# The weighing's last tile of 64 keys a head: one fp32 product, or three products of split fp32r halves

## The reference

```python
def _attn_ref(q, k, v, cap):
    scores = np.matmul(q, k.transpose(0, 1, 3, 2)) / np.sqrt(q.shape[-1])
    scores = cap * np.tanh(scores / cap)
    attn = np.exp(scores - np.max(scores, axis=-1, keepdims=True))
    attn = attn / (np.sum(attn, axis=-1, keepdims=True) + 1e-09)
    return np.matmul(attn, v)

h = x @ w_in
x = np.maximum(0.01 * h, h) @ w_out
xn = x / np.sqrt(np.mean(x * x, axis=-1, keepdims=True) + 1e-06) * rms_g
g = xn @ w_gate
out = (g / (1 + np.exp(-g)) * (xn @ w_val)) @ w_out2
```

## Time and profile before

| what | value |
|---|---|
| runs before (3) | 567.91 us median, 567.53 to 568.76 |
| the profiled execution's own time | 568.21 us |
| its span | 566.4 us |
| TensorE busy | 561.6 us (99%) |
| VectorE busy | 413.7 us (73%) |
| ScalarE busy | 294.4 us (52%) |
| GpSimd busy | 313.8 us (55%) |

### The profile page before, as it was taken

One profiled execution on the slowest core, in us unless ns is written; L12 is line 12 of the kernel. 1 busy time (PEld: TensorE's weight loads), 2 busy tenths in 40 slices (PEclk: granted clock), 3 DMA queues, 4 the chain that ended last, 5 costly groups with the idle time before them and its releaser, 6 DMA issues.

```text
span 566.4 us, 7857 instructions
## 1 busy us (share of the span) xinstructions
PE 561.6 (99%) x2706; PEld 472.0 (83%) x2706; DVE 413.7 (73%) x575; ACT 294.4 (52%) x513; POOL 313.8 (55%) x272
## 2 busy tenths in 40 slices
PE   9999999999999999999999999999999999999997
PEld 5544554688999999999999999999999999998896
DVE  4468897685545455324985499999999999999963
ACT  6889888226444464434644456444334445825330
POOL 1026464479656652234853469767766897526672
PEclk9999999999999999999999999999999999999999
DMA  6355332123111142110211011111221111120511
GB/s 171 97 174 162 110 113 52 49 57 112 57 56 57 56 130 66 57 45 23 75 54 57 1 57 57 56 57 56 77 89 59 56 57 58 56 57 0 171 73 65
DMA packets 29720, 41.49 MB, mean 73 GB/s; under 512 B 17009, under 2 KB 18673, under 8 KB 29681
## 3 DMA queue, kind: packets, MB, share of 16 engines
q1 hardware_dynamic: 29536, 40.99, 23.0%
q10 hardware_dynamic: 144, 0.00, 0.0%
HBM read 38.15 MB, written 2.80 MB: 72 GB/s over the span
## 4 chain that ended last, share of the span: by engine, by line
PE 91%; DVE 4%; issue 3%; DMA 1%; ACT 0%; POOL 0%; DVEq 0%; ACTq 0%
PE ps L1579 46%; PE ps L1646 21%; PE ps L1514 9%; PE ps L1743 8%; PE ps L1502 4%; PE ps L1520 2%; PE ps L1506 1%; DVE act_lo L1321 1%; DVE x_lo L1321 1%; PE ps L1588 1%; DMA sums<-x_raw 1%; DVE x_raw L955 0%; DVE s_sum L1024 0%; POOL w_lo L576 0%; PE ps L1698 0%
## 5 line engine op out<-in xcount | busy, mean ns | idle before, releaser
L576 POOL TENSOR_TENSOR w_lo<-w_raw,w_hi 128x384 fp32r<-128x384 f32 x111 | 131.1, 1189 | 140.3 <-ACT w_hi L686 139.6
L1579 PE MATMUL ps<-x_hi,w_hi 128*128 128x448 f32 x420 | 154.9, 369 | 0.0
L1579 PE MATMUL ps<-x_hi,w_lo 128*128 128x448 f32 x420 | 154.1, 367 | 0.0
L1579 PE MATMUL ps<-x_lo,w_hi 128*128 128x448 f32 x420 | 154.0, 367 | 0.0
L576 POOL TENSOR_TENSOR w_lo<-s_sum,w_hi 128x384 fp32r<-128x384 f32 x100 | 113.6, 1149 | 69.5 <-ACT w_hi L686 69.5
L686 ACT ACTIVATE w_hi<-s_sum 128x384 fp32r<-128x384 f32 x100 | 51.2, 523 | 91.6 <-PE ps L1579 53.3
L1579 PEld LDWEIGHTS ps<-x_hi,w_hi 128*128 128x128 f32 x420 | 79.0, 188 | 8.4 <-issue 1.3
L1579 PEld LDWEIGHTS ps<-x_hi,w_lo 128*128 128x128 f32 x420 | 78.9, 188 | 7.0
L1579 PEld LDWEIGHTS ps<-x_lo,w_hi 128*128 128x128 f32 x420 | 79.0, 188 | 6.7
L686 ACT ACTIVATE w_hi<-w_raw 128x384 fp32r<-128x384 f32 x111 | 56.3, 514 | 11.8 <-PE ps L1579 7.2
L1514 PE MATMUL ps<-probs,v_ones 128*65 128x448 f32 x144 | 56.6, 541 | 0.2 <-DVE x_raw L955 0.2
(11 more groups left out here) (182 smaller groups left out, 1047.2 us busy)
## 6 DMA issues: line engine op xcount, KB each, us to landing
w_raw<-in_w_out SPq DMA_DIRECT2D x28, 384.0 KB, 3.1
w_raw<-in_w_in SPq DMA_DIRECT2D x16, 384.0 KB, 3.8
qk_raw<-in_qk SPq DMA_DIRECT2D x11, 480.0 KB, 4.3
w_raw<-in_w_gate SPq DMA_DIRECT2D x12, 384.0 KB, 3.0
w_raw<-in_w_val SPq DMA_DIRECT2D x12, 384.0 KB, 3.6
v_ones<-in_v SPq DMA_DIRECT2D x12, 224.0 KB, 3.3
recip_row<-recips SPq DMA_DIRECT2D x12, 224.0 KB, 3.3
out<-sq SPq DMA_DIRECT2D x6, 224.0 KB, 1.9
```

Source lines behind the costliest of these rows:

```text
L576: pool.tensor_tensor(w_lo[:, c], source, w_hi[:, c].bitcast(F32), ALU.subtract).then_inc(w_lo_done, 1)
L1579: last = pe.matmul(ps[:, base(s) + BANK_OF[j], 0:S], w[:, w_c], x[:, xs(j, c)], start=(j in (P1, P5, P7, P6) and c == 0 and w is w_hi and ...
```

## The change

The weighing of the tile of 64 keys is done in the split form. ScalarE makes the upper half of the pair's 448 last probabilities (`rest_hi`, a copy to fp32r) right behind the exp that ends the pair. GpSimd makes the lower half of the probabilities (`rest_lo`) and both halves of v's 64 + 2 columns (`v_rest_hi`, `v_rest_lo`), in a new function `split_rest` that stands at the head of its round. `weigh_rest` becomes three fp32r products a head in place of one fp32 product, behind waits for the four new semaphores. All products of the weighing take 66 columns of v instead of 65; what they write into the 66th row is not read. The halves of the probabilities lie where `p1`, `a_t` and `u2` lie later.

```diff
+        v_rest_hi = [buf(f"v_rest_hi{s}", D + 2, F32R) for s in range(2)]
+        v_rest_lo = [buf(f"v_rest_lo{s}", D + 2, F32R) for s in range(2)]
+        at(P1_AT)
+        rest_hi = [buf(f"rest_hi{s}", S, F32R) for s in range(2)]
+        at(U2_AT)
+        rest_lo = [buf(f"rest_lo{s}", S, F32R) for s in range(2)]
...
+            def split_rest(p):
+                at_least(pool, pv_done, p - 1)
+                pool.wait_ge(v_in[p % 2], 16 * (p // 2 + 1))
+                pool.tensor_copy(v_rest_hi[p % 2][:, :], v_rest(p)).then_inc(v_rest_hi_done, 1)
+                pool.wait_ge(v_rest_hi_done, p + 1)
+                pool.tensor_tensor(v_rest_lo[p % 2][:, :], v_rest(p), v_rest_hi[p % 2][:, :].bitcast(F32),
+                                   ALU.subtract).then_inc(v_rest_lo_done, 1)
+                pool.wait_ge(rest_hi_done, p + 1)
+                pool.tensor_tensor(rest_lo[p % 2][:, :], rest_probs(p), rest_hi[p % 2][:, :].bitcast(F32),
+                                   ALU.subtract).then_inc(rest_lo_done, 1)
+
             for p in range(PAIRS):
+                split_rest(p)
                 if 0 <= p - 3 < 7:
                     weight_lo(p - 3)
...
                 exp(p, 1 + int(p == 0))
+                act.wait_ge(exp_done, exps_before(p + 1))
+                act.activation(rest_hi[p % 2][:, :], rest_probs(p), ACT.Copy).then_inc(rest_hi_done, 1)
                 if 0 <= p - 3 < 7:
                     weight_hi(p - 3)
...
             def weigh_rest(p):
-                c = 2 * MAIN * 128
-                for h in range(2):
-                    last = pe.matmul(ps[0:D + 1, pv_bank(p) + h, 0:S], v_ones[p % 2][HEAD[h], c:c + D + 1],
-                                     probs[p % 2][HEAD[h], 2 * MAIN * S:(2 * MAIN + 1) * S], start=False, stop=True)
+                pe.wait_ge(v_rest_lo_done, p + 1)
+                for v_part, x in ((v_rest_hi, rest_hi), (v_rest_hi, rest_lo), (v_rest_lo, rest_hi)):
+                    if x is rest_lo:
+                        pe.wait_ge(rest_lo_done, p + 1)
+                    elif v_part is v_rest_hi:
+                        pe.wait_ge(rest_hi_done, p + 1)
+                    for h in range(2):
+                        last = pe.matmul(ps[0:D + 2, pv_bank(p) + h, 0:S], v_part[p % 2][HEAD[h], :], x[p % 2][HEAD[h], :],
+                                         start=False, stop=(v_part is v_rest_lo))
                 last.then_inc(pv_done, 1)
```

More of the change, by code:

```diff
@@ L112, in build @@
         w_lo = buf("w_lo", 7 * HALF, F32R)
+        P1_AT = place["at"]
         p1 = [buf(f"p1_{s}", S, F32) for s in range(2)]
         a_t = [buf(f"a_t{s}", S, F32) for s in range(2)]
+        U2_AT = place["at"]
         u2 = [buf(f"u2_{s}", S, F32) for s in range(2)]
@@ L191, in build @@
         exp_done = sem("exp_done")
+        v_rest_hi_done = sem("v_rest_hi_done")
+        v_rest_lo_done = sem("v_rest_lo_done")
+        rest_hi_done = sem("rest_hi_done")
+        rest_lo_done = sem("rest_lo_done")
         pv_done = sem("pv_done")
@@ L282, in probs_of, with rest_probs, v_rest @@
             return probs[p % 2][:, 2 * i * S:(2 * i + n) * S]
+        def rest_probs(p):
+            return probs[p % 2][:, 2 * MAIN * S:(2 * MAIN + 1) * S]
+        def v_rest(p):
+            return v_ones[p % 2][:, 2 * MAIN * 128:2 * MAIN * 128 + D + 2]
         def xs(blk, c):
@@ L1513, in weigh_tile @@
                     c = (h * MAIN + t) * 128
-                    pe.matmul(ps[0:D + 1, pv_bank(p) + h, 0:S], v_ones[p % 2][:, c:c + D + 1],
+                    pe.matmul(ps[0:D + 2, pv_bank(p) + h, 0:S], v_ones[p % 2][:, c:c + D + 2],
                               probs[p % 2][:, (2 * t + h) * S:(2 * t + h + 1) * S], start=(t == 0), stop=False)
             def weigh_rest(p):
-                c = 2 * MAIN * 128
-                for h in range(2):
-                    last = pe.matmul(ps[0:D + 1, pv_bank(p) + h, 0:S], v_ones[p % 2][HEAD[h], c:c + D + 1],
-                                     probs[p % 2][HEAD[h], 2 * MAIN * S:(2 * MAIN + 1) * S], start=False, stop=True)
+                pe.wait_ge(v_rest_lo_done, p + 1)
[7 more added lines that the diff above has]
+                                         start=False, stop=(v_part is v_rest_lo))
                 last.then_inc(pv_done, 1)
```

## The result

The changed kernel takes 571.57 us (median of 4 runs, 571.07 to 572.37) against 567.86 us (567.53 to 568.76): a ratio of 1.0064, 95% interval 1.0048 to 1.0080. It is slower by 3.7 us. The profiled execution took 572.37 us, the longest of its four.

The account below looks back on a forecast made before the run. TensorE bounds the attention, with VectorE's rounds 0.1 us behind; GpSimd's new work takes turns with VectorE. VectorE's 8.1 us later, less 1.0 of air and 0.4 saved by TensorE, gives 6.7: 574.6 us, range 571.2 to 577.8.

Parts of the forecast that it names:

- The signs: Trace marks of a right forecast: keep_x(9) near 98.7, ordinary VectorE stretches near 5.4 us, stretched L961 and `normalise`, TensorE waiting for keep_x.
- TensorE's gain, 0.10 a pair: In `weigh_rest`: 0.90 us becomes 0.80, so 1.2 us over 12 pairs; by the other row 0.29 a pair, 3.5 us.
- ScalarE, nothing: The copy `rest_hi`, 0.57 us a piece, fits in ScalarE's 0.87 us of waiting a pair and costs nothing.
- GpSimd, 1.5 us a pair: New GpSimd work per pair: `rest_lo` 1.16, `v_rest_lo` by columns 0.2, `v_rest_hi` 0.1 to 0.15, together 1.5 us.
- Who takes turns with whom: After keep_x, VectorE and GpSimd alternate whole SBUF instructions; L961 stands behind `rest_lo`, `normalise` behind `w_lo`; 5.4 us a round.
- The size, 8.1 us on VectorE: Seven stretches from keep_x to the end of `normalise` grow from 30.93 to 39.0 us, making keep_x(9) later by 8.1.
- The air: Slack taken off VectorE's lateness: 0.7 us in round 6, 0.1 before pair 10, 0.2 from an earlier keep_x(2).
- Behind the attention: Nothing after the attention takes the loss back; a turn for `rest_lo(11)` could add a wait of up to 0.8 us.
- (a): Rival: the turns do not bite in VectorE's rounds, TensorE gains up to 1.2 us: 566.7, or 564.4 with 0.29; chance 0.07.
- (b): Rival: nothing to measure, half the turns hit and DMA waits cover them, within 1.1 us of 567.9; chance 0.05.
- (c): Rival: TensorE waits inside `weigh_rest` for `rest_lo`, 577 to 579 us; chance 0.1.
- (d): Rival: ScalarE becomes the bound, TensorE waiting 0.2 us a pair for its copy, 2.4 in all: 570.3; chance 0.03.

Follow-up runs that it names:

- e3: The changed kernel without `rest_lo`, TensorE multiplying the upper half twice in its place; v's two small GpSimd instructions stay: 567.06 against 567.04 us, ratio 0.9996.
- e6: The changed kernel with GpSimd's `rest_lo` made twice, the second behind the first: 579.17 against 567.80 us, ratio 1.0195.
- e1: The changed kernel with the fp32 product put back into `weigh_rest`, the split work on ScalarE and GpSimd still made: 572.15 against 567.04 us, ratio 1.0082.
- e2: The kernel before plus ScalarE's copy `rest_hi`, which nobody reads, and 66 columns of v; nothing new on GpSimd: 567.99 against 567.04 us, ratio 1.0004.
- e9: The changed kernel, unchanged, measured and traced again: 573.39 against 566.70 us, ratio 1.0109.
- e5: The kernel before, unchanged, run once more for a second trace: 566.15 us in one run, span 564.4.
- e10: The changed kernel's three products on upper halves only, v's made by ScalarE, nothing new on GpSimd or VectorE: 567.14 against 566.70 us, ratio 1.0000.
- e4: The kernel before with an added TensorE wait ahead of the third part of x in its first feed-forward product: 568.39 against 567.04 us, ratio 1.0014.
- e7: The changed kernel with `rest_lo` made by VectorE behind `split_qk` instead of by GpSimd: 570.42 against 567.80 us, ratio 1.0049.
- e8: The changed kernel with GpSimd's `weight_lo` of rounds 3 to 9 moved to later rounds: 571.61 against 567.80 us, ratio 1.0061.
- e12: The changed kernel with v's upper half on ScalarE, both lower halves on VectorE, weights moved later, nothing new on GpSimd: 568.88 against 566.70 us, ratio 1.0029.

## Why the prediction was right, point by point

The forecast was 574.6 us, 6.7 above before; measured were 3.7 and, again, 6.7 above. The mechanism is shown: e3 takes away `rest_lo` and the loss is gone, e6 doubles it and the loss grows by 4.7 to 7.7, e1 and e2 clear the new products and ScalarE. The size is in part luck. The first measurement lies only 0.4 above the lower end of the range of 571.2 to 577.8; and in the sum a term that was too large stands beside one that was left out, as shown below.

- **The signs.** TensorE's waits at the head of `weigh` name VectorE's keep_x, 5.1 us. The stretch to the end of `normalise` is 5.12 in rounds 4 and 8. L994 takes 0.98 to 0.99 in three rounds. The rounds did not stay at 8.5: three of them, 68.57 to 96.29, take 9.24 each. One sign failed: keep_x(9) starts at 96.29 (96.39 in e9) and not near 98.7.
- **TensorE's gain, 0.10 a pair.** Measured 0.14, nearer to this than to the 0.29 of the other row. From start to start the six products take 0.67, between the 0.61 of one row and the 0.80 of the other: 0.26 for the first two behind the weighing, then 0.20 and 0.21. The six at 10.96 had 128-row products behind them too, and these six do not.
- **ScalarE, nothing.** Right: 0.58 a copy, e2 within 0.2%.
- **GpSimd, 1.5 us a pair.** Alone: 0.24 and 0.33 for v's halves, 1.13 for `rest_lo`, 1.7 together.
- **Who takes turns with whom.** In the rounds 4, 6 and 8 the walk came as written: L994 0.99 behind `rest_lo`, `normalise` 1.91 behind `w_lo`. In 3, 5 and 9 the first instruction of `normalise` had its turn before `rest_lo` and the second stood behind it (2.04, 2.19 and 2.19 for both), and `w_lo` met `combine`. In round 7 `normalise` met `rest_lo` and `w_lo`, 2.80. The Trainium skill, SBUF — State Buffer, section "SBUF: two separate sides", speaks of an exclusive lock; the trace agrees, the 0.17 of L994 becoming 0.99.
- **Two readings of the trace before.** That the turns of L994, the cast and L995 fit to the hundredth is no test, because 0.42 and 0.49 are what was left over; alone such a cast takes 0.56 (at 108.52 in e5) and such a sum 0.63. And that `w_lo` cost nothing before holds for round 4. In the other rounds it had already stretched VectorE: L961 took 0.33 to 0.95 in 3, 5, 6 and 9, and `normalise` 1.84 and 1.89 in 7 and 8.
- **The size, 8.1 us on VectorE.** This is the term that was mis-sized. The stretches are 35.21 and not 39.0: 5.0 to 5.3 in six rounds against 5.4 and 6.0, and 4.50 in round 3. Of the 3.8 too much, 1.9 sit where the prediction chose 6.0, in rounds 5 and 9 (5.05 and 5.03, from 4.85 and 4.84): with x's splitting still in the way, v's halves and `rest_lo` added only 0.2 there and pushed `w_lo` out into `combine`. Another 0.9 is round 3, where v's halves had been made before keep_x(2) (30.72 and 31.44) and `w_lo` fell behind `normalise`, so that the stretch has two instructions of GpSimd in it and not four. The last 1.0 is spread over the other four; in round 4 the small cast cost nothing, since `qk_lo` takes its 1.16 as before, and L994 was done 0.02 after `rest_lo`, where 0.2 had been counted. On the other side stand three stretched instructions of `combine`, 2.1 us, of which the prediction had nothing. Together the rounds grew by 62.60 - 56.97 = 5.6 us; between the traces of equal pace, e9 and e5, by 62.91 - 57.45 = 5.5.
- **The air.** Round 6 lost its 0.71 of waiting for TensorE in this 5.6 already, so the rest of the rounds grew by 6.3, which is the 4.3 of the stretches and the 2.1 of `combine`. keep_x(2) started 1.3 us earlier than in the first trace of before, because the weights landed earlier; between e9 and e5 it is 0.5.
- **Behind the attention.** The first feed-forward product comes 4.45 later in e9 than in e5 (109.02, 104.57); the wait for the third part of x adds 0.5, and the spans differ by 5.0 (569.4, 564.4). The forecast allowed that wait up to 0.8; in the first trace it was 1.34. There, too, it is a turn behind `rest_lo(11)`: L994 of the last round took 1.05 in the first trace, and in e9 `normalise` took 2.05 instead of 1.23.
- **The rivals.** (a) and (b), turns that don't bite: refuted by the stretched rows and by e6. (c), TensorE held by `rest_lo`: no such wait in the changed kernel, 3.6 us in e6. (d), ScalarE: refuted by e2. And e10 shows that the gain of (a) would not have come: with no new turn at all nothing was gained.

That the first measurement shows 3.7 and the second 6.7 is more than their intervals allow for one number. Two things that differ between executions are seen in the traces, the pace of the first feed-forward stage (up to 2.2 us) and the landing of the first weights (up to 3 us, of which a part reaches the end); that they make the whole difference is not shown, nor is what decides either of them. The 5.0 of the traces of equal pace, one trace of each kernel on two different chips, is the best value that the record has for the change itself.

## What to carry to other kernels

An idle engine is not free if its instructions and those of a busy one take turns, as GpSimd's and VectorE's do here on SBUF. Ask of each instruction that it is given what the other would be doing at that time, and walk both programs in turns; here the cost landed on the engine that was given nothing. And before a product is made shorter, see who releases its engine next: here VectorE's rounds stood 0.1 us behind TensorE, so that the shorter product alone (e10) was worth nothing. Where a change is worth less than 1%, take a second trace of the kernel before, and compare traces whose long untouched stages run at the same pace.

## What was not expected of the hardware

- Products of 448 columns in fp32r start every 0.2036 us in one execution and every 0.2076 us in another of the same kernel, through a whole stage of 504, at a granted clock of 1.00 in both (e5 and the first trace of before). It moves the end of that stage by 1.7 us. The 14 traces fall into three groups: 0.2036 to 0.2042 in seven, 0.2066 to 0.2069 in five (e4, e6, e7, e8, e12), 0.2076 and 0.2079 in two (the first of before, e10).
- VectorE's first sum of weights waits for a DMA that landed at 32.0 in e2, 32.6 in the changed kernel, 33.4 in e5, 34.5 in the first trace of before and 35.1 in e12. No edit touches that load: it was issued at 28.2 in the first trace of before and at 28.4 in the changed kernel, and took 6.2 and 4.2 us to land. The rounds of VectorE start by it. It goes with the pace: in the seven traces of the fastest pace the sum starts at 32.0 to 33.4, in the seven others at 33.3 to 35.1. Why is open.
- A subtraction of 66 columns on GpSimd takes 0.33 us alone and 1.20 when VectorE has the turn; the price of a small instruction is mostly its place.
